# TensorE broadcasts of all first scales, a new startup and weight-loading order, and a deeper lag in the last block of a fused mLSTM and two-layer MLP kernel

## The reference

```python
for t in range(S):
    m_new = np.maximum(f_gate[:, :, t] + m, i_gate[:, :, t])
    f_stab = np.exp(f_gate[:, :, t] + m - m_new)
    i_stab = np.exp(i_gate[:, :, t] - m_new)
    C = f_stab * C + i_stab * outer(vt, kt)
    n = f_stab * n + i_stab * kt
    y[:, :, t] = sigmoid(o_gate[:, :, t]) * (C @ qt) / np.maximum(np.abs(n @ qt), 1.0)
x = y.transpose(0, 2, 1, 3).reshape(B * S, H * D)
x = leaky(x @ moe_w_in) @ moe_w_out          # leaky(h) = max(0.01 h, h)
out = (lambda h: h * np.cos(h))(x @ moe2_w_in) @ moe2_w_out
```

## Time and profile before

| | |
|---|---|
| time, median of 3 runs | 835.13 us (834.86 to 835.85) |
| the profiled execution: its own time | 836.9 us |
| the profiled execution: its span | 835.1 us |
| TensorE busy | 815.9 us, 98% of the span |
| VectorE, ScalarE, GpSimd busy | 76%, 56%, 41% |
| DMA, mean | 84 GB/s |

### The profile page before, as it was taken

How to read it: one execution, slowest core, us unless ns; L and a number is a source line. 1 busy time by engine, 2 the same in 40 slices (tenths; PEclk the granted TensorE clock), 3 DMA queues, 4 the chain that set the end, 5 groups by cost and what they waited for, 6 DMA issues and landing times.

```text
span 835.1 us, 18267 instructions
## 1 busy us (share of the span) xinstructions
PE 815.9 (98%) x6953; PEld 784.8 (94%) x6953; DVE 633.1 (76%) x1377; ACT 465.3 (56%) x1033; POOL 339.9 (41%) x350
## 2 busy tenths in 40 slices
PE   8789999999999999999999999999999999999997
PEld 6678899999999999999999999999999999999997
DVE  7679677677677866777853588888888888888886
ACT  5245443433433434334336687767776767777776
POOL 5656534343333433433316643333333333333332
PEclk9989999999999999999999999999999999999999
DMA  9555522423444324235023410302020202020000
GB/s 300 174 151 149 172 78 79 126 78 82 129 134 131 89 79 125 79 91 183 1 96 108 121 75 2 119 2 72 1 72 1 72 1 71 1 72 1 20 5 25
DMA packets 37292, 70.26 MB, mean 84 GB/s; under 512 B 3544, under 2 KB 24408, under 8 KB 37208
## 3 DMA queue, kind: packets, MB, share of 16 engines
q1 hardware_dynamic: 36708, 68.86, 26.7%
q10 hardware_dynamic: 500, 0.26, 0.1%
HBM read 57.11 MB, written 11.99 MB: 83 GB/s over the span
## 4 chain that ended last, share of the span: by engine, by line
PE 90%; DVE 4%; ACT 1%; DMA 1%; issue 1%; POOL 1%; SPq 1%; DVEq 0%; POOLq 0%; ACTq 0%
PE h L635 32%; PE acc L647 13%; PE acc L649 13%; PE acc L648 13%; PE s L635 10%; PE x L613 2%; PE s L593 2%; PE s L577 2%; PE s L605 2%; PE s L558 1%; DVE g_lo L1194 1%; DMA raw_in<-w1i 1%; DVE kvo_s L1073 1%; DMA eG_b<-e_dram 1%; ACT t_f L791 0%
## 5 line engine op out<-in xcount | busy, mean ns | idle before, releaser
L635 PE MATMUL h<-xT,w_in 128*128 128x384 f32 x1536 | 306.5, 341 | 0.5 <-DVE xT L1186 0.5
L635 PEld LDWEIGHTS h<-xT,w_in 128*128 128x128 f32 x1536 | 266.5, 188 | 3.6 <-DVE xT L1186 0.6
L791 ACT ACTIVATE t_f<-h 128x384 f32<-128x384 f32 x192 | 94.4, 492 | 291.9 <-PE h L635 291.8
L647 PE MATMUL acc<-w_out,g_hi 128*128 128x320 f32 x768 | 242.1, 315 | 2.2 <-POOL g_lo L1533 1.8
L649 PE MATMUL acc<-w_out,g_lo 128*128 128x320 f32 x768 | 237.5, 309 | 0.0
L648 PE MATMUL acc<-w_out,g_hi 128*128 128x320 f32 x768 | 236.2, 308 | 0.0
L1533 POOL TENSOR_TENSOR g_lo<-g_f,g_hi 128x384 fp32r<-128x384 f32 x127 | 130.2, 1025 | 211.9 <-ACT g_hi L791 211.9
L1207 DVE TENSOR_TENSOR g_f<-h,t_f 128x384 f32<-128x384 f32 x128 | 71.2, 556 | 105.7 <-ACT t_f L791 105.7
L647 PEld LDWEIGHTS acc<-w_out,g_hi 128*128 128x128 f32 x768 | 144.6, 188 | 4.6 <-POOL g_lo L1533 2.0
L648 PEld LDWEIGHTS acc<-w_out,g_hi 128*128 128x128 f32 x768 | 144.7, 188 | 0.0
L649 PEld LDWEIGHTS acc<-w_out,g_lo 128*128 128x128 f32 x768 | 144.3, 188 | 0.0
(11 more groups left out here) (150 smaller groups left out, 792.5 us busy)
## 6 DMA issues: line engine op xcount, KB each, us to landing
qk_s<-qk SPq DMA_DIRECT2D x24, 512.0 KB, 3.8
kvo_s<-kvo SPq DMA_DIRECT2D x24, 484.0 KB, 5.2
x_dram<-stage SPq DMA_DIRECT2D x8, 960.0 KB, 6.0
xT<-x_dram SPq DMA_DIRECT2D x8, 960.0 KB, 4.9
D<-g_dram SPq DMA_DIRECT2D x42, 128.0 KB
qe<-q SPq DMA_DIRECT2D x24, 160.0 KB, 5.5
out<-x SPq DMA_DIRECT2D x24, 160.0 KB, 1.8
eG_b<-e_dram SPq DMA_DIRECT2D x42, 80.0 KB
```

The source lines that it names most:

```text
L635: last = nc.tensor.matmul(bank[:, 0:BLOCK], w(a), x[:, k, :], start=(n == 0), stop=(n == 7))
L647: nc.tensor.matmul(acc[t][:, 0:DM], g_hi[:, s, r], w_out[:, 0, j, :], start=(j == 0), stop=False)
L791: copy = lambda o, i, **k: nc.scalar.activation(o, i, ACT.Copy, **k)
```

## The change

1. `spread_scales`, `first_scales` and the waits serve unit 2 too, through the bank x; `store_scales` moves to SyncE's queue and `load_scales` is gone. VectorE clears 384 instead of 256 columns of `keep_all`, twice.
2. TensorE makes unit 2's scores, scales and state before the outputs of units 0 and 1; VectorE and GpSimd are reordered with it.
3. SyncE's order for block 0 changes: e store 0 is there, piece 3's input weights are issued before the wait for the stores, the decays of unit 4 go behind q3 and kvo (0,5), those of unit 5 behind piece 4's input weights. GpSimd takes the rest of input piece 1 ahead of `second_columns`.
4. In the last block (tiles 240 to 255) the ring has six places: two are made of xT and kvo_s, both free by then. Slots 4 and 9 of that block issue no second product, so the lag grows to 4 and then 5 tiles; after the last first product come the second products of tiles 10 (in slot 15), 11 and 12, 13 and 14, and 15.

```diff
@@ -41,6 +41,8 @@
 RING = 4
+DEEP = 6
+SKIPS = (4, 9)
 BUFS = 3
@@ -122,6 +124,9 @@
         GH = BATCH * HEADS
+        more_hi, more_lo = xT[:, 0, 0:DEEP - RING, :], xT[:, 0, DEEP - RING:2 * (DEEP - RING), :]
+        more_f = kvo_s[:, 0, 0:(DEEP - RING) * BLOCK].rearrange("p (s t) -> p s t", s=DEEP - RING)
@@ -235,7 +240,7 @@
-            return (b * (CHUNKS // BUFS) + c // BUFS) * DECAY_DMAS * 16 + (DECAY_DMAS // 2 * 16 if c % BUFS == 2 else 0)
+            return (b * (CHUNKS // BUFS) + c // BUFS) * DECAY_DMAS * 16
@@ -329,6 +334,30 @@
         TILES_TOTAL = 2 * BLOCKS * FT
+        LAST = TILES_TOTAL - FT
+        def slot_of(tile):
+            return (tile - LAST) % DEEP if isinstance(tile, int) and tile >= LAST else tile % RING
+        def slot_before(tile):
+            users = [t for t in range(tile - 2 * DEEP, tile) if slot_of(t) == slot_of(tile)]
+            return users[-1] if tile >= LAST and users else tile - RING
+        def in_ring(ring, more, tile):
+            s = slot_of(tile)
+            return ring[:, s, :] if s < RING else more[:, s - RING, :]
+        def hi_of(tile):
+            return in_ring(g_hi, more_hi, tile)
+        def lo_of(tile):
+            return in_ring(g_lo, more_lo, tile)
+        def g_of(tile):
+            return in_ring(g_f, more_f, tile)
@@ -433,6 +462,8 @@
             load_q3(0, 3)
+            sp.wait_ge(gate_exp, 1)
+            store_gates(e_dram, keep[:, 0:TILES, :], 0).then_inc(e_stored, 16)
             wait_count(S_done, 3)
@@ -441,24 +472,24 @@
             store_gates(g_dram, G_s[1].rearrange("p (c t) -> p c t", c=TILES), 1).then_inc(scratch, 16)
+            wait_count(x1_done, 2)
+            load_kvo(0, 4)
+            load_raw_in(w1i, 2)
             sp.wait_ge(gate_exp, 3)
             store_gates(e_dram, keep[:, TILES:CHUNKS, :], 1).then_inc(scratch, 16)
-            sp.wait_ge(x1_done, 2)
-            load_kvo(0, 4)
-            load_raw_in(w1i, 2)
-            load_raw_out(w1o, 2)
+            load_raw_in(w1i, 3)
             sp.wait_ge(scratch, 32)
...
             load_unit_decays(0, 3)
-            load_unit_decays(0, 4)
-            load_raw_in(w1i, 3)
-            load_raw_out(w1o, 3)
-            sp.wait_ge(x1_done, 3)
+            load_raw_out(w1o, 2)
+            wait_count(x1_done, 3)
             load_q3(0, 5)
             load_kvo(0, 5)
+            load_unit_decays(0, 4)
+            load_raw_out(w1o, 3)
+            load_raw_in(w1i, 4)
             load_unit_decays(0, 5)
-            load_raw_in(w1i, 4)
             load_raw_out(w1o, 4)
@@ -528,7 +559,7 @@
         def scale_bank(c):
-            return (h_bank[0], acc[0])[c]
+            return (h_bank[0], acc[0], x_bank)[c]
@@ -636,7 +667,8 @@
             def second_product(row, i):
-                s, j = i % RING, i % FT
+                j = i % FT
+                hi, lo = hi_of(row.tile(i)), lo_of(row.tile(i))
                 pe.wait_ge(lo_done, row.tile(i) + 1)
...
@@ -696,8 +728,7 @@
                     turn_columns(i_s, 0, 0)
-                if i >= LAG:
-                    o = i - LAG
+                for o in seconds(row, i):
                     if row.starts(0, o) and o % PT == 0:
@@ -708,6 +739,21 @@
                     unit_within(*u)
+            def seconds(row, i):
+                if i < LAG:
+                    return []
+                j = row.tile(i) - LAST
+                if j < SKIPS[0]:
+                    return [i - LAG]
+                if j in SKIPS:
+                    return []
+                skipped = sum(j > k for k in SKIPS)
+                if j < FT:
+                    return [i - LAG - skipped]
+                rest = [i - j + k for k in range(FT - LAG - skipped, FT)]
+                return rest[(j - FT) * 2:(j - FT) * 2 + 2] if j < FT + LAG - 1 else rest[(j - FT) * 2:]
@@ -765,15 +811,16 @@
             unit_state(0, 1)
-            unit_carried(0, 0)
-            unit_within(0, 0)
             spread_decays(2)
...
             unit_scores(0, 2)
+            pe.wait_ge(cols_done, 1)
+            spread_scales(2)
             unit_state(0, 2)
+            unit_carried(0, 0)
+            unit_within(0, 0)
             unit_carried(0, 1)
             unit_within(0, 1)
-            pe.wait_ge(dx_done, TILES)
             warm_up(WARM[1], acc[2])
@@ -809,18 +856,6 @@
-            def store_scales():
-                act.wait_ge(gate_exp, 1)
-                nc.scalar.dma_start(e_dram[0:TILES].rearrange("c b h t -> (b h) c t"), keep[:, 0:TILES, :]).then_inc(e_stored, 16)
-            def load_scales(c):
-                act.wait_ge(e_stored, 16)
-                for i in range(PACK):
-                    x = e_dram[c, 0:1, i::PACK]
-                    nc.scalar.dma_start(eG_b[HD * i:HD * (i + 1), c, :, :], x.to_broadcast([HD, GROUPS, CHUNK])).then_inc(decays_in[c], 16)
             def first_state():
@@ -859,8 +894,8 @@
             def g_round(row, i):
-                act.wait_ge(out_done, (row.tile(i) - RING + 1) * TILES + OUT_FREE)
-                copy(g_hi[:, i % RING, :], g_f[:, i % RING, :]).then_inc(hi_done, 1)
+                act.wait_ge(out_done, (slot_before(row.tile(i)) + 1) * TILES + OUT_FREE)
+                copy(hi_of(row.tile(i)), g_of(row.tile(i))).then_inc(hi_done, 1)
...
@@ -984,7 +1019,6 @@
             gate_scale(0)
-            store_scales()
             gate_weights(0)
@@ -994,10 +1028,10 @@
             first_scales(1)
-            load_scales(2)
             sigmoid_exp(0, 2)
...
             first_decays(2)
+            first_scales(2)
             split_out_hi(0)
@@ -1023,7 +1057,7 @@
                 nc.vector.memset(i_all[r, :], 0.0).then_inc(blank_done, 1)
-                nc.vector.memset(keep_all[r, 0:2 * CHUNK], 0.0).then_inc(blank_done, 1)
+                nc.vector.memset(keep_all[r, 0:TILES * CHUNK], 0.0).then_inc(blank_done, 1)
@@ -1154,10 +1188,7 @@
                 if first(b, c):
-                    if c < 2:
-                        dve.wait_ge(eG_done, c + 1)
-                    else:
-                        dve.wait_ge(decays_in[c], decays_loaded(b, c))
+                    dve.wait_ge(eG_done, c + 1)
                 for u in range(SUBS if c < CHUNKS - 1 else 1):
...
@@ -1291,14 +1322,14 @@
             state(0, 1)
+            sigmoid(0, 1, 1)
+            first_probs(2)
+            sigmoid(0, 2, 0)
+            state(0, 2)
             normaliser(0, 0)
-            first_probs(2)
-            sigmoid(0, 1, 1)
-            state(0, 2)
+            sigmoid(0, 2, 1)
             normaliser(0, 1)
-            sigmoid(0, 2, 0)
             outputs(0, 0)
-            sigmoid(0, 2, 1)
             outputs(0, 1)
@@ -1403,10 +1434,7 @@
-                if c < 2:
-                    pool.wait_ge(eG_done, c + 1)
-                else:
-                    pool.wait_ge(decays_in[c], decays_loaded(0, c))
+                pool.wait_ge(eG_done, c + 1)
                 carried(0, c)
@@ -1496,9 +1524,10 @@
             split_in_lo(0)
+            pool.wait_ge(G_done, 2)
+            split_in_lo(1)
             second_columns()
             split_out_lo(0)
-            split_in_lo(1)
             split_out_lo(1)
...
```

More of the change, by code:

```diff
@@ L646, in second_product @@
                         pe.wait_ge(acc_read, row.block(i) * TILES + t + 1)
-                    nc.tensor.matmul(acc[t][:, 0:DM], g_hi[:, s, r], w_out[:, 0, j, :], start=(j == 0), stop=False)
-                    nc.tensor.matmul(acc[t][:, 0:DM], g_hi[:, s, r], w_out[:, 1, j, :], start=False, stop=False)
-                    nc.tensor.matmul(acc[t][:, 0:DM], g_lo[:, s, r], w_out[:, 0, j, :], start=False,
+                    nc.tensor.matmul(acc[t][:, 0:DM], hi[:, r], w_out[:, 0, j, :], start=(j == 0), stop=False)
+                    nc.tensor.matmul(acc[t][:, 0:DM], hi[:, r], w_out[:, 1, j, :], start=False, stop=False)
+                    nc.tensor.matmul(acc[t][:, 0:DM], lo[:, r], w_out[:, 0, j, :], start=False,
                                      stop=(j == FT - 1)).then_inc(out_done, 1)
@@ L876, in rounded @@
                     act.wait_ge(prod_done, done + PROD_FREE + c)
-                    copy(g_hi[:, i % RING, c * P:(c + 1) * P], g_f[:, i % RING, c * P:(c + 1) * P]).then_inc(hi_done, 1)
+                    copy(hi_of(row.tile(i))[:, c * P:(c + 1) * P], g_of(row.tile(i))[:, c * P:(c + 1) * P]).then_inc(hi_done, 1)
                 for c, r in thirds(r_f[:, i % 2, :]):
@@ L1193, in g_rest @@
                 dve.wait_ge(hi_done, row.tile(i) + 1)
-                tt(g_lo[:, i % RING, :], g_f[:, i % RING, :], g_hi[:, i % RING, :].bitcast(F32), ALU.subtract).then_inc(lo_done, 1)
+                tt(lo_of(row.tile(i)), g_of(row.tile(i)), hi_of(row.tile(i)).bitcast(F32), ALU.subtract).then_inc(lo_done, 1)
             def slot(row, i):
@@ L1206, in slot @@
                     dve.wait_ge(lin_done, row.tile(i) + 1)
-                    tt(g_f[:, i % RING, :], h_bank[i % 2][:, 0:BLOCK], t_f[:, i % 2, :], ALU.max).then_inc(max_done, 1)
```

(11 more changed lines are left out.)

## The result

The changed kernel takes **831.07 us** (median of five, 829.89 to 832.88) against 835.51 in the same measurement; the ratio is 0.9947, with a 95% interval of 0.9931 to 0.9963. So it is faster by 4.4 us, not by 11. A second measurement of it gave 831.20 (829.96 to 833.06) against 836.64, ratio 0.9939 (0.9922 to 0.9955). The profiled execution is the fastest of its five, 829.89, with a span of 828.1: 7.0 less than the span of the profiled execution of before. Both the 7.0 and the 4.4 need explaining.

What follows compares the result with a forecast made beforehand. TensorE was taken as the bound, busy 815.9 of 835.1 us; terms -2.6 - 3.4 - 2.4 - 2.6 = -11.0 took 836.9 to 825.9, and 1.8 off for the median gave 824.1. Own range 822.3 to 825.8; 8 in 10 range to 829.0.

Steps and rivals of the forecast that it cites:

- Part 1, -2.6: Startup: unit 2's state comes earlier, so the first MLP tile starts at 33.5 instead of 36.07, 2.6 us less.
- I work GpSimd out to 27.15: Startup: GpSimd finishes its list before unit 1's gated output at 27.15, against 26.6 on VectorE, a wait of 0.55 us.
- 9.4 - 1.07 + 0.75 + 0.55: Startup: time from unit 2's `state` to the end of x1, taken as 10.0 us with rounding.
- they cost nothing while VectorE is behind: Startup: eight added TensorE passes to spread the scales, like those of 1.10 us, replace dummy matmuls and cost nothing.
- Part 2, -3.4 and -2.4: Block 0: TensorE's long wait goes, 3.4 us less, and the slow clock behind it goes, 2.4 us less.
- what is late next: Block 0: the decays of unit 3 come next; P is ready at 44.4, TensorE there at 45.9, slack 1.5 us.
- I cost these at nothing, covered by that slack: Block 0: the other reordered loads and GpSimd's earlier `split_in_lo` cost nothing, within 1.5 us of slack.
- the fast rows: Block 0: earlier stores that landed in 1.6 us; by them the e store lands at 33.2, slack 2.8 us.
- The rival of a new wait: Block 0: decays or a weight piece come 3 to 4 us too late; 829.9, or 827 if short; chance 0.15.
- Part 3, -2.6: Last block: two skipped second products let the last first product end 2.64 us earlier; 2.6 us less in time.
- The overlap stays as it is: Last block: VectorE's reductions slide no further under GpSimd's g_lo, since both distances are fixed work.
- the condition reckoned 0.36 a tile: Last block: VectorE must catch up 2.64 us from its idle 0.36 per tile, four tiles for each 1.32.

Runs made afterwards that it cites:

- f1: Changed kernel, but GpSimd's masked copy of unit 1's second state no longer waits for unit 0's output: 828.49 us, ratio 0.9920.
- e2: Kernel before with the startup part alone: 835.24 us against 835.39, ratio 0.9995.
- g3: Kernel before without its first five dummy matmuls at the start: 835.64 us against 835.67, ratio 1.0001.
- f2: Changed kernel with the second e store ahead of kvo (0,4) and input piece 2 on SyncE's queue: 831.15 us, ratio 0.9938.
- f4: Changed kernel with the edits of f1, f2 and f3 together: 829.54 us, ratio 0.9928.
- g1: Kernel of f1, with both sigmoid halves of a unit behind its state on VectorE in block 0: 830.32 us, ratio 0.9924.
- e1: Kernel before with the last block's part alone (six places, two skipped second products): 833.56 us against 835.39, ratio 0.9975.
- f3: Changed kernel with three more dummy matmuls in TensorE's idle stretch before the first decays: 829.89 us, ratio 0.9925.

## Why the prediction was wrong

The prediction was wrong: 824.1 was forecast, with a range to 829.0, and it is 831.07.

**Part 1, -2.6.** The step "I work GpSimd out to 27.15" failed: it took `own_state` of unit 1 as ready with its input, and passed over its wait for unit 0's output, which the change moves back. It is the very question to ask of a moved step: who waits for what was moved. Its price is 1.4 to 1.5 us (f1 gets it back and lands on 33.44). The memsets cost their 0.2 (first decays 6.63 to 6.90), and `state` started at 21.47. That f1 lands so near 33.5 is in part luck: the terms 9.4 - 1.07 + 0.75 + 0.55 give 9.6, which the text calls 10.0 with rounding, and in f1 VectorE waits 0.88 us for GpSimd's `gated`, not 0.55, which fills just that gap.

**Part 1, the condition.** The step "they cost nothing while VectorE is behind" treats TensorE's time as given. Startup's clock was nowhere in the sum. The change takes a wait for DRAM out of a chain that could hide some 2 us of slow TensorE; then TensorE's speed is on the path. On the median the part alone is worth nothing (e2).

**Part 2, -3.4 and -2.4.** The mechanism was right: piece 3 left early, and the wait and the dip behind it went. The sizes were those of one execution. Its wait was 3.39, others with the same order had 2.51, 2.51 and 2.88, and from the first tile to the last block it took 756.2 us, they 754.8 to 755.7. Its granted clock was 0.996, while 17 of 30 executions of the kernel before had 0.998 and ten 0.996; in g3, at 0.998, the dip to 0.50 lasted 3.4 us, in this one 6.8. Those at 0.996 took 835.4 to 837.3 us, those at 0.998 833.4 to 836.0. So I took the gain from an execution 1.8 us above the median and then took the 1.8 off the result again. Taking the terms off that execution's own time is right for a total, but a term that removes a variable wait must be priced at its usual size.

**Part 2, "what is late next".** "I cost these at nothing, covered by that slack" failed. The store took 3.9 us, not 2.9; the ring-order rule of the Trainium skill (DMA: Bandwidth & Descriptors, section "Queues, rings and completion order") was nearer than the fast rows: the store behind two large loads took 3.9, in f2 ahead of them 1.6. But f4 and g1 show that it did not matter much. VectorE had no idle time from 40 to 52 us, and neither the product P nor the state behind it could be early. I had followed the decays and never laid out VectorE's list in block 0. New waits of 0.94, 1.22 and 0.55 came, less a 0.37 that went: 2.3 us. The rival of a new wait had the place right and the price too high.

**Part 3, -2.6.** Right in kind, too large by 0.5: it is 2.1 (2.11 in the changed kernel, 2.08 in e1). The step "The overlap stays as it is" failed: without its idle 0.36 VectorE slid further under g_lo, and the reduction went from 0.91 to 1.18. The rule of the Trainium skill that I had set beside it (GPSIMD Engine Reference, section "Specifications") was the one to follow: this trace agrees with it. VectorE had to catch up 2.64. It gained 0.44 on the tile before the deeper overlap (2.29 us from 789.96 to 792.25, instead of 2.73) and 0.19 on each of the ten behind it (2.54 a tile), 2.4 in all, where the condition reckoned 0.36 a tile; and its last tile took 0.25 longer than before. By the 0.19 a tile, skips four tiles later would have left it 0.8 us less; no run shows that.

**The sum.** 1.14 + 3.76 + 2.11 is the 7.0 between the two profiled executions. From 7.0 to 4.4 is the choice of executions: before's was above its median by 1.4, the changed kernel's below its own by 1.2. What stays open is how often the clock rises late in each kernel, since only the timelines of profiled executions show it and the granted clock does not; what makes it rise late in one execution and early in a like one; and what the waits of block 0 are at the median.

## What to carry to other kernels

When a step is moved back, look up everyone who waits for it, also through a counter with an offset that looks settled, and write out the full list of the busiest engine in the stage, not only the chain of what was late. Taking a transfer out of a chain puts on the path what the transfer had been hiding; here it was TensorE's speed in the first 11 us, and three dummy matmuls won back 1.2 us at the median (f3), where the new startup alone had won nothing (e2). Price a variable wait from several executions, or say that there is only one. And measure a part between two marks that lie close around it: counted from tile 10 the last block seemed worth 2.5, counted from its own start it was 2.1 in every trace.
